# Attention with an MLP behind it: transposes one step later, inverse sums as rows through memory, first weights ahead of the last sums

## The chip, the cores and the metric

One core of a Trainium2 chip. The metric is device time of one execution in microseconds (us), the median of three runs: 931.72 before the change (931.66 to 932.09).

## What is computed

```python
q_pool = q.reshape(B, H, S // 2, 2, D).mean(axis=3)      # B 4, H 8, S 1152, D 64
scores = matmul(q_pool, k.transpose(0, 1, 3, 2)) / sqrt(D)
scores = scores - max(scores, axis=-1)
attn = exp(scores)
attn = attn / (sum(attn, axis=-1) + 1e-09)
x = matmul(attn, v)            # then to (B * S/2 tokens = 2304, H * D = 512)
h = x @ w_in                   # 512 x 2048
g = maximum(h, 0) + alpha * minimum(h, 0)
out = g @ w_out                # 2048 x 512
```

All of it in float32. The MLP's products are made of three: high by high, low by high and high by low part.

## The kernel before

**Attention.** The 32 heads are taken as 16 pairs; the two heads of a pair have 2 x 576 pooled queries, which are 9 tiles of 128 (`SOURCE`; tile 4, `MIX`, is half from either head). So there are 144 steps, one tile each, and `step` is written once for each engine; `t` is the tile's number in its pair. `over_steps` runs the first steps out by hand, then seven loop bodies of 18 steps (two pairs), then the rest. A step s does, in the order of each engine's own queue:

- PE: 16 small transposes (L587) of the first 1024 key columns of tile s's exponentials into two banks, `slot_ps`; the big scores of tile s+2 (L532, 1024 key columns); the ninth transpose (L547, the last 128 key columns) and the small scores of tile s+2 (L520), both in the middle bank of `s_ps`; then a part of the product with v (L573), of 2 to 6 matmuls. The product is made in two groups of tiles (`GROUPS`: 320 columns of tiles 0 to 4, 256 of tiles 5 to 8) and spread over later steps (`PRODUCT`). In step 6 and in step 1 a spread stands ahead of the product.
- ACT: exponential of the cut 128 columns of tile s+1 (L341), copy of slot 0 into `pt` (L357), exponential of the other 1024 columns of tile s+1 (L348). Both exponentials write their row sums, which shows as an accumulator read behind them.
- DVE: copy of slot 1 (L465), copy of the ninth block (L472), row maximum of tile s+2 (L432). In steps 4 and 8 it inverts the row sums of a group (`INVERT`), in steps 0 and 5 it scales a group's product by them (L440), and in step 5 it casts the pair's x to its high part (L446), from which POOL makes the low part (L287).
- SP: loads of q, k and v two pairs ahead, each behind a semaphore that says that its buffer is free. POOL sums pairs of q rows.

What the engines wait for in a step: PE's transposes for the exponential of tile s (`exp_done`) and for both slots (`slot_free`); the ninth transpose for its copy-out (`ninth_free`) and for the cut exponential of tile s+1 (`exp_cut_done`), which reads the same bank; DVE's ninth copy and row maximum for the small scores (`bank2_ready`, `s_ready`); ACT's cut exponential for the row maximum.

The row sums lie one query a partition, and the product has its queries along the columns. `spread_inverse` gets them there on PE: a matmul of the inverse, broadcast over 64 columns, with the identity writes it as a row into 64 partitions, piece by piece into slot 0:

```python
last[h] = nc.tensor.matmul(to[h * D:(h + 1) * D, col[h]:col[h] + m],
                           inv_sum[:, t:t + 1].to_broadcast([P, D]),
                           ident[:, first:first + m], start=True, stop=True)
```

ACT copies that to `inv_bc` (L363) and frees the slot.

**MLP.** Three passes over 768 tokens each, in two halves h of 384; 16 blocks f of 128 hidden units a pass. `hidden_unit` is 12 matmuls (L617), `output_unit` 9 (L632), in two halves in turn: hidden(f, 1), output(f, 0), hidden(f+1, 0), output(f, 1). Between them DVE forms the sum g of a half in two instructions (L479, L482), ACT casts it to its high part (L404, L415), DVE subtracts for the low part (L488). ACT casts the weights, POOL subtracts for theirs (`wi_split`, `wo_split`), SP loads them. `x_hi` and `x_lo` hold all of x in both parts. The first hidden unit comes before the last pair's second product group and its spread.

## Time and profile before

| | before |
|---|---|
| median of 3 runs | 931.72 us |
| the profiled execution | 932.26 us, its span 929.70 us |
| PE, busy of the span | 887.3 us (95%) |
| PE weight loads | 623.2 us (67%) |
| DVE | 516.9 us (56%) |
| ACT | 423.4 us (46%) |
| POOL | 213.3 us (23%) |
| attention, first step to the MLP's first matmul | 19.6 to 515.9 us |
| MLP | 515.9 to 929.7 us |

Busy shares are means over both stages. Matmuls are pipelined and their ends are modelled, so a row of PE can be busy while PE waits; starts are what they are. A span is counted from the first instruction to the last; the execution's own time has 2.56 us around it.

### The profile page before, as it was taken

Reading aid. Unit: us, or ns where it says so; the run is one execution under the profiler, and the core shown is the slowest. Engines: PE = TensorE matmul, PEld = TensorE weight load, DVE = VectorE, ACT = ScalarE, POOL = GpSimd, SP = SyncE. Lnnn points to the kernel's source line nnn. Section 1 sums busy time; section 2 is a strip of 40 time slices with the busy share of each in tenths; the row PEclk is TensorE's granted clock in tenths of the full one; section 3 lists DMA queues with packets and bytes.
Section 4 is the critical chain, followed back from the end, with each engine's and each line's share of the span. In section 5 each row is a group of like instructions: output and inputs, shape, how many; then the busy total and the mean of one; then the engine's idle time right before and its main releaser. Section 6 shows DMA issues by size and latency. Waiting matters only on the chain. (4 is left out here: it accounts for less than half of the span.)

```text
span 929.7 us, 20770 instructions
## 1 busy us (share of the span) xinstructions
PE 887.3 (95%) x6896; PEld 623.2 (67%) x6896; DVE 516.9 (56%) x836; ACT 423.4 (46%) x963; POOL 213.3 (23%) x182
## 2 busy tenths in 40 slices
PE   3799999999999999999999999999999999999997
PEld 1455555555555555555545799989999999989995
DVE  2676767677767776767676344344444444343442
ACT  2566666666666666666666222222322222322222
POOL 2112111211121112111200323323232323323230
PEclk9999999999999999999999999999999999999999
DMA  7435423542354235523520122212422222322211
GB/s 186 106 83 135 119 65 82 133 121 63 82 133 123 60 82 133 127 57 82 133 71 1 59 68 58 67 62 63 136 57 68 57 68 61 132 59 66 65 36 68
DMA packets 36366, 79.57 MB, mean 86 GB/s; under 512 B 5360, under 2 KB 9456, under 8 KB 36336
## 3 DMA queue, kind: packets, MB, share of 16 engines
q1 hardware_dynamic: 33936, 74.48, 31.0%
q10 hardware_dynamic: 2400, 4.72, 1.5%
q8 instruction: 16, 0.26, 0.1%
q14 instruction: 14, 0.11, 0.0%
HBM read 74.46 MB, written 4.72 MB: 85 GB/s over the span
## 5 line engine op out<-in xcount | busy, mean ns | idle before, releaser
L432 DVE TENSOR_REDUCE neg_max<-s_ps 128x1 f32<-128x1152 f32 x144 | 194.1, 1348 | 16.6 <-DVEq L431 16.6
L573 PE MATMUL pv_ps<-pt,v_f 128*64 128x256 f32 (+1 forms) x1152 | 169.0, 414 | 0.0
L532 PE MATMUL s_ps<-k_f,q_f 64*128 64x512 f32 (+1 forms) x640 | 160.2, 626 | 5.2 <-PEq L543 5.2
L348 ACT ACTIVATE e_sb<-s_ps,neg_max 128x1024 f32<-128x1024 f32 x144 | 160.1, 1112 | 0.0
L587 PEld LDWEIGHTS slot_ps<-ident,e_sb 64*128 64x128 f32 x2304 | 86.0, 139 | 82.4 <-issue 82.4
L465 DVE COPY pt<-slot_ps 128x512 f32<-128x512 f32 x144 | 99.6, 692 | 61.3 <-DVEq L464 59.4
L341 ACT ACTIVATE e_sb<-s_ps,neg_max 128x128 f32<-128x128 f32 x144 | 52.9, 367 | 171.5 <-ACTq L340 171.5
L617 PE MATMUL slot_ps<-x_hi,wi_hi 128*128 128x384 f32 x384 | 129.5, 337 | 1.1 <-PEq L613 1.1
L617 PE MATMUL slot_ps<-x_lo,wi_hi 128*128 128x384 f32 x384 | 129.5, 337 | 0.0
L617 PE MATMUL slot_ps<-x_hi,wi_lo 128*128 128x384 f32 x384 | 129.0, 336 | 0.0
L479 DVE TENSOR_SCALAR e_sb<-slot_ps,alpha_sb 128x384 f32<-128x384 f32 x96 | 59.3, 618 | 123.2 <-DVEq L477 123.2
L587 PE MATMUL slot_ps<-ident,e_sb 64*128 64x64 f32 x2304 | 103.5, 229 | 18.6 <-PEq L582 15.4
L488 DVE TENSOR_TENSOR g_lo<-e_sb,g_hi 128x384 fp32r<-128x384 f32 x96 | 53.7, 559 | 99.6 <-DVEq L487 99.6
L573 PEld LDWEIGHTS pv_ps<-pt,v_f 128*64 128x64 f32 x1152 | 73.5, 136 | 40.1 <-issue 0.2
L632 PE MATMUL s_ps<-wo_lo,g_hi 128*128 128x512 f32 x240 | 95.1, 396 | 0.0
L632 PE MATMUL s_ps<-wo_hi,g_lo 128*128 128x512 f32 x240 | 94.8, 395 | 0.0
L547 PEld LDWEIGHTS s_ps<-ident,e_sb 128*128 128x128 f32 x144 | 19.9, 138 | 111.5 <-issue 111.4
L632 PE MATMUL s_ps<-wo_hi,g_hi 128*128 128x512 f32 x240 | 93.4, 389 | 1.1 <-PEq L629 1.1
L303 POOL TENSOR_TENSOR wo_lo<-wo_raw,wo_hi 128x512 fp32r<-128x512 f32 x48 | 61.9, 1290 | 138.5 <-POOLq L302 138.5
L272 POOL TENSOR_TENSOR q_raw<-q_raw 128x576 f32<-128x576 f32 x32 | 45.0, 1406 | 209.7 <-POOLq L271 209.7
L404 ACT ACTIVATE g_hi<-e_sb 128x384 fp32r<-128x384 f32 x48 | 25.3, 526 | 148.9 <-ACTq L403 148.9
L295 POOL TENSOR_TENSOR wi_lo<-wi_raw,wi_hi 128x512 fp32r<-128x512 f32 x48 | 61.8, 1287 | 135.6 <-POOLq L294 135.6
(46 smaller groups left out, 1098.8 us busy)
## 6 DMA issues: line engine op xcount, KB each, us to landing
q_raw<-in_q SPq DMA_DIRECT2D x64, 288.0 KB, 4.5
k_f<-in_k SPq DMA_DIRECT2D x64, 288.0 KB, 4.2
wi_raw<-in_w_in SPq DMA_DIRECT2D x48, 256.0 KB, 2.6
wo_raw<-in_w_out SPq DMA_DIRECT2D x48, 256.0 KB, 2.6
v_f<-in_v SPq DMA_DIRECT2D x32, 288.0 KB, 3.0
out<-pt ACTq DMA_DIRECT2D x6, 768.0 KB, 4.4
k_end<-in_k SPq DMA_DIRECT2D x64, 32.0 KB, 4.0
alpha_sb<-in_alpha SPq DMA_DIRECT2D x1, 8.0 KB, 4.7
```

The lines of the kernel that those rows point to most:

```text
L295: nc.gpsimd.tensor_tensor(wi_lo[i][:, :], wi_raw[i][:, :], wi_hi[i][:, :].bitcast(F32), ALU.subtract).then_inc(pool_self, 1)
L303: nc.gpsimd.tensor_tensor(wo_lo[i][:, :], wo_raw[i][:, :], wo_hi[i][:, :].bitcast(F32), ALU.subtract).then_inc(pool_self, 1)
L348: nc.scalar.activation(e_sb[:, b * NKEY + at:b * NKEY + at + n], s_ps[:, S_AT[b] + at:S_AT[b] + at + n], ACT.Exp, bias=neg_max[:, b:b + 1] ...
L432: nc.vector.tensor_reduce(out=neg_max[:, b:b + 1], in_=s_ps[:, S_AT[b]:S_AT[b] + NKEY], op=ALU.max, axis=AX_X, negate=True).then_inc(max_r ...
L465: nc.vector.tensor_copy(pt_half(t, 1), half_columns(slot_ps[1][:, :])).then_inc(slot_free[1], 1)
L479: nc.vector.tensor_scalar(neg_sb, hid, 0.0, alpha_sb[:, bass.ds(f, 1)], ALU.min, ALU.mult).then_inc(dve_self, 1)
L488: nc.vector.tensor_tensor(g_lo[h][:, :], g_sb, g_hi[h][:, :].bitcast(F32), ALU.subtract).then_inc(g_split, 1)
L532: ins = nc.tensor.matmul(s_ps[to:to + m, S_AT[b] + at:S_AT[b] + at + BANK], q_f[2 * g + h][rows, first:first + m], k_f[2 * g + h][rows, at ...
L573: ins = nc.tensor.matmul(pv_ps[h * D:(h + 1) * D, 0:n], v_f[2 * g + h][:, a, :], pt[:, a, at:at + n], start=(a == 0), stop=(a == KT - 1))
L587: ins = nc.tensor.transpose(slot_ps[i][:, a * HALF:(a + 1) * HALF], e_sb[rows, at:at + P], ident[rows, rows])
L617: ins = nc.tensor.matmul(slot_ps[h][:, 0:TOK], w[i][:, d * P:(d + 1) * P], x[:, at:at + TOK], start=(d == 0 and w is wi_hi and x is x_hi), ...
L632: ins = nc.tensor.matmul(y_ps[h][t], g[h][:, t * P:(t + 1) * P], w[i][:, :], start=(first == 0 and j == 0), stop=(last == 1 and j == 2))
```

## The change

1. *Transposes.* Step s transposes tile s-1 (the 16 small ones and the ninth) instead of tile s. The exponentials get a third buffer in `e_sb`. PE's wait for `exp_done` stands now behind the transposes, ahead of the big scores, and the waits ahead of the ninth transpose are `exp_cut_done` first, `ninth_free` second. One step is added at the end. `PRODUCT` and `INVERT` move one step later.
2. *Inverse sums.* `spread_inverse` goes. PE transposes the [128 x 5] or [128 x 4] inverses into 5 or 4 rows in the middle bank (`turn_inverse`, in steps 6 and 1, between ninth transpose and small scores), DVE copies them to `inv_row` (between ninth copy and row maximum), SP stores them to a tensor `sums` in device memory and, when that has landed, loads them with a broadcast into 64 partitions twice, to `inv_bc`. DVE scales in steps 1 and 6, the first thing in its step. The order of queries in a pair changes so that the rows come in one piece (`SOURCE`, `SUM_AT`, `PT_AT`).
3. *x.* DVE writes the scaled product to `x_f`, all of x in float32. High and low parts are made for a half pass: the first two by POOL (`x_split`) before the MLP, the others at the end of a pass by ACT (`x_high`) and DVE (`x_low`).
4. *Weights.* The first cast of w_in stands in ACT's last step but one, ahead of the last slot copy; SP loads the first four weight blocks before it stores and spreads the last pair's sums.

The core of the diff:

```diff
 def step(s, pair, left=2):                      # PE
-    pe.wait_ge(exp_done, 1).then_inc(exp_done, -1)
-    for i in range(2):
-        pe.wait_ge(slot_free[i], 1).then_inc(slot_free[i], -1)
-    for a in range(2 * CH):
-        at = s % 2 * NKEY + a * P
+    if s > 0:
+        for i in range(2):
+            pe.wait_ge(slot_free[i], 1).then_inc(slot_free[i], -1)
+        for a in range(2 * CH):
+            at = (s - 1) % 3 * NKEY + a * P
...
+    if left >= 0:
+        pe.wait_ge(exp_done, 1).then_inc(exp_done, -1)
     if left > 1:
         begin_scores(s + 2)
         for ins in big_scores(s + 2):
             ins.then_inc(s_ready, 1)
-    pe.wait_ge(ninth_free, 1).then_inc(ninth_free, -1)
     if left > 0:
         pe.wait_ge(exp_cut_done, 1).then_inc(exp_cut_done, -1)
-    ins = transposed(s, 2 * CH, NINTH)
+    if s > 0:
+        pe.wait_ge(ninth_free, 1).then_inc(ninth_free, -1)
+        ins = transposed(s - 1, 2 * CH, NINTH)
+    if t in TURN and (TURN[t] == 0 or pair is not None):
+        ins = turn_inverse(TURN[t])
     if left > 1:
         ins = small_scores(s + 2)
     ins.then_inc(bank2_ready, 1)
...
-        if t in SPREAD:
-            pe.wait_ge(slot_free[0], 1).then_inc(slot_free[0], -1)
-            spread_inverse(SPREAD[t], slot_ps[0])
...
+def turn_inverse(group):
+    a, b = GROUP_TILES[group]
+    pe.wait_ge(inv_ready, 1).then_inc(inv_ready, -1)
+    return nc.tensor.transpose(INV_ROW[0:b - a, :], inv_sum[:, a:b], ident[:, :])
...
+def sums_and_qk(pair, g):                       # SP
+    store_sums(0)
+    load_q(pair * 2)
+    spread_sums(0)
+    sp.wait_ge(k_free[g], 1).then_inc(k_free[g], -1)
+    load_k(pair * 2, 2 * g), load_k(pair * 2 + 1, 2 * g + 1)
+    store_sums(1)
+    load_q(pair * 2 + 1)
+    spread_sums(1)
...
+def store_sums(group):
+    a, b = GROUP_TILES[group]
+    sp.wait_ge(inv_row_ready, 1).then_inc(inv_row_ready, -1)
+    sp.dma_start(sums[a * P:b * P].rearrange("(t p) -> t p", p=P),
+                 inv_row[0:b - a, :]).then_inc(inv_stored, 16)
+def spread_sums(group):
+    _, _, n, first = GROUPS[group]
+    sp.wait_ge(inv_stored, 16).then_inc(inv_stored, -16)
+    for h in range(2):
+        row = sums[GROUPS[group][h]:GROUPS[group][h] + n]
+        sp.dma_start(inv_bc[h * D:(h + 1) * D, first:first + n],
+                     row.rearrange("(o n) -> o n", o=1).to_broadcast([D, n])).then_inc(inv_bc_in[group], 16)
...
 def hidden(f, i, first, last):                  # ACT, end of a pass
     act.wait_ge(g_ready, 1).then_inc(g_ready, -1)
     nc.scalar.activation(g_hi[0], g_sb, ACT.Copy).then_inc(g_hi_done, 1)
+    if last and not last_pass:
+        x_high(n + 1, 0)
...
 def hidden(f, i, first, last):                  # DVE
     unit(f, 0)
     if n == 0 and not first:
-        scale(1)
-        x_high(NPAIR - 1)
+        scale(1, NPAIR - 1)
+    if last and not last_pass:
+        x_low(0)
     unit(f, 1)
+    if last and not last_pass:
+        x_low(1)
```

How the instructions move. First PE's queue in steps 0 and 1 of a pair, inside the loop (L587 and L631 are the small transposes, L532 and L586 the big scores, L547 and L601 the ninth transpose, L520 and L574 the small scores, L573 and L617 the product; L557 the spread, L606 the new transpose of the inverses). Before:

```order
L587 MATMUL slot_ps<-ident,e_sb 128x64 [waits exp_done,slot0_free,slot1_free]
L587 MATMUL slot_ps<-ident,e_sb 128x64 x15
L532 MATMUL s_ps<-k_f,q_f 128x512 x2
L547 MATMUL s_ps<-ident,e_sb 128x128 [waits ninth_free,exp_cut_done]
L520 MATMUL s_ps<-k_end,q_f 128x128
L557 MATMUL slot_ps<-ident,inv_sum 64x128 [waits slot0_free,inv_ready]
L557 MATMUL slot_ps<-ident,inv_sum 64x128 x3
L573 MATMUL pv_ps<-pt,v_f 64x256 x4
```

After:

```order
L631 MATMUL slot_ps<-ident,e_sb 128x64 [waits slot0_free,slot1_free]
L631 MATMUL slot_ps<-ident,e_sb 128x64 x15
L586 MATMUL s_ps<-k_f,q_f 128x512 [waits exp_done]
L586 MATMUL s_ps<-k_f,q_f 128x512
L601 MATMUL s_ps<-ident,e_sb 128x128 [waits exp_cut_done,ninth_free]
L606 MATMUL s_ps<-ident,inv_sum 4x128 [waits inv_ready]
L574 MATMUL s_ps<-k_end,q_f 128x128
L617 MATMUL pv_ps<-pt,v_f 64x256 [waits pv_free]
L617 MATMUL pv_ps<-pt,v_f 64x256 x3
```

The wait for the exponential has moved from the transposes to the big scores, the two waits ahead of the ninth transpose have changed places, and one transpose with a wait of its own stands where the spread's four matmuls stood behind the small scores (of the step before and after the same number, 1).

On DVE, step 6 after (L479 is the scale, L506 and L513 slot and ninth copy, L496 the copy of the inverse rows, L471 the row maximum); before, step 6 had L465, L472 and L432 alone:

```order
L479 ISA [waits inv_bc1_in,pv_done]
L479 TENSOR_TENSOR x_f<-pv_ps,inv_bc 128x256
L506 COPY pt<-slot_ps 128x8x64 [waits x_self,tr1_ready]
L513 COPY pt<-s_ps 128x128 [waits bank2_ready]
L496 COPY inv_row<-s_ps 5x128
L471 TENSOR_REDUCE neg_max<-s_ps 128x1 [waits s_ready]
```

The scale heads the step, and its wait holds the copies and the maximum behind it.

On SP, the first group of loads for a later pair after (L217 and L218 load q, L221 k, L237 stores the inverse rows, L246 loads them spread); before, the q and k loads stood there alone:

```order
L237 DMA sums<-inv_row 5x128 [waits inv_row_ready]
L217 DMA q_raw<-in_q 64x1152 [waits q_raw_free]
L218 DMA q_raw<-in_q 64x1152
L246 DMA inv_bc<-sums 64x320 [waits inv_stored]
L246 DMA inv_bc<-sums 64x320
L221 DMA k_f<-in_k 64x1152 [waits k0_free]
```

The loads of q stand between the store and the spread, and those of k behind both waits.

## Rows read from the trace of the kernel before

**Rows 1.** Windows by stage: us, busy us (x instructions) per engine, clock, DMA share, GB/s
```profile
19.60:52.60 33.00, 27.07 (x264) 14.54 (x263) 21.91 (x32) 19.01 (x46) 6.23 (x6) 0.95 0.53 128
52.60:485.20 432.60, 419.87 (x4274) 224.57 (x4272) 305.45 (x476) 273.62 (x658) 75.72 (x68) 1.00 0.40 99
485.20:515.90 30.70, 27.87 (x296) 15.22 (x294) 19.65 (x33) 19.62 (x46) 2.70 (x3) 1.00 0.00 1
515.90:929.70 413.80, 407.02 (x2060) 366.85 (x2060) 167.42 (x290) 108.34 (x208) 123.85 (x96) 1.00 0.24 70
```

**Rows 2.** List of waits, PE: us in total, times, longest us
```profile
PE slot_ps L587 <- PEq L582: 15.4, 35, 1.4
```

**Rows 3.** Timeline, PE: transposes of steps 0-3, 6-8, 0: start us, length us
```profile
299.77 0.71 PE L587 MATMUL slot_ps<-ident,e_sb 64*128 64x64 f32 x16
302.83 0.71 PE L587 MATMUL slot_ps<-ident,e_sb 64*128 64x64 f32 x16
306.59 0.71 PE L587 MATMUL slot_ps<-ident,e_sb 64*128 64x64 f32 x16
309.75 0.71 PE L587 MATMUL slot_ps<-ident,e_sb 64*128 64x64 f32 x16
...
319.69 0.71 PE L587 MATMUL slot_ps<-ident,e_sb 64*128 64x64 f32 x16
323.57 0.71 PE L587 MATMUL slot_ps<-ident,e_sb 64*128 64x64 f32 x16
326.84 0.71 PE L587 MATMUL slot_ps<-ident,e_sb 64*128 64x64 f32 x16
330.65 0.71 PE L587 MATMUL slot_ps<-ident,e_sb 64*128 64x64 f32 x16
```

**Rows 4.** Timeline: end of step 4's exponential and its transposes
```profile
312.62 0.21 ACT L348 ACTIVATION_READ_ACCUMULATOR e_sb<-s_ps,neg_max 128x1 f32 x1
313.27 0.71 PE L587 MATMUL slot_ps<-ident,e_sb 64*128 64x64 f32 x16 [0.35 <-PEq L582]
```

**Rows 5.** Timeline: one turn of the ninth block, step 2 to step 3
```profile
308.25 0.33 PE L547 MATMUL s_ps<-ident,e_sb 128*128 128x128 f32 x1
309.11 0.29 DVE L472 COPY pt<-s_ps 128x128 f32<-128x128 f32 x1 [0.96 <-DVEq L471]
309.32 1.35 DVE L432 TENSOR_REDUCE neg_max<-s_ps 128x1 f32<-128x1152 f32 x1
...
310.79 0.37 ACT L341 ACTIVATE e_sb<-s_ps,neg_max 128x128 f32<-128x128 f32 x1 [1.70 <-ACTq L340]
311.05 0.19 ACT L341 ACTIVATION_READ_ACCUMULATOR e_sb<-s_ps,neg_max 128x1 f32 x1
311.39 0.30 PE L547 MATMUL s_ps<-ident,e_sb 128*128 128x128 f32 x1
312.06 0.29 DVE L472 COPY pt<-s_ps 128x128 f32<-128x128 f32 x1 [0.72 <-DVEq L471]
```

**Rows 6.** Timeline, PE: the spread of step 1
```profile
304.95 0.66 PE L557 MATMUL slot_ps<-ident,inv_sum 128*64 128x128 f32 x8
```

**Rows 7.** Timeline, DVE: scale and slot copy of step 5
```profile
317.00 0.41 DVE L440 TENSOR_TENSOR x_sb<-pv_ps,inv_bc 128x256 f32<-128x256 f32 x1
317.86 0.69 DVE L465 COPY pt<-slot_ps 128x512 f32<-128x512 f32 x1 [0.44 <-DVEq L464]
```

**Rows 8.** DMA issues: count, KB each, median us from issue to landing
```profile
q_raw<-in_q SPq DMA_DIRECT2D x64, 288.0 KB, 4.5
wi_raw<-in_w_in SPq DMA_DIRECT2D x48, 256.0 KB, 2.6
```

**Rows 9.** Timeline: one MLP sum on DVE, with ACT's cast
```profile
525.12 0.62 DVE L479 TENSOR_SCALAR e_sb<-slot_ps,alpha_sb 128x384 f32<-128x384 f32 x1 [1.15 <-DVEq L477]
526.80 0.53 ACT L415 ACTIVATE g_hi<-e_sb 128x384 fp32r<-128x384 f32 x1 [5.69 <-ACTq L414]
527.48 0.56 DVE L488 TENSOR_TENSOR g_lo<-e_sb,g_hi 128x384 fp32r<-128x384 f32 x1 [1.03 <-DVEq L487]
```

More of the change, by code:

```diff
@@ L13, with build @@
 BANK = 512
-def build(nc, q, k, v, w_in, w_out, alpha, out):
+def build(nc, q, k, v, w_in, w_out, alpha, sums, out):
     HEADS, D, NKEY = k.shape
@@ L138, in build @@
         inv_ready = sem("inv_ready")
[L139 to L140 removed]
+        inv_row_ready = sem("inv_row_ready")
+        inv_stored = sem("inv_stored")
+        inv_bc_in = [sem(f"inv_bc{i}_in") for i in range(2)]
         pv_done = sem("pv_done")
         pv_free = sem("pv_free")
[L143 removed]
+        x_done = sem("x_done")
         x_hi_done = sem("x_hi_done")
@@ L178, in over_steps, with x_chunk, x_part @@
                     step(s, two * 2)
-            for s in range(FIRST, REST):
+            for s in range(FIRST, REST + 1):
                 step(s, 2 * BODIES, REST - 1 - s)
+        def x_chunk(n, h):
+            at = (2 * n + h) * TOK
+            return x_f[:, :].rearrange("p (d c) -> p d c", d=DT)[:, :, at:at + TOK]
+        def x_part(part, h):
+            return part[h].rearrange("p (d c) -> p d c", d=DT)
         def pt_half(t, half):
-            at = PT_AT[t] if half == 0 else PT_MIX if t == MIX else PT_AT[t] + HALF
+            at = PT_AT[t] + half * HALF
             return pt[:, 0:2 * CH, at:at + HALF]
@@ L443, in scale @@
                 dve.sem_inc(pv_free, 1)
-            def x_high(pair):
-                nc.vector.tensor_copy(x_hi[:, bass.ds(pair * NQ, NQ)], x_sb[:, :]).then_inc(x_hi_done, 1)
+                if group == 1:
+                    dve.sem_inc(x_done, 1)
             def invert(group):
@@ L507, in hidden @@
                     if n == 0 and not first:
-                        scale(1)
-                        x_high(NPAIR - 1)
+                        scale(1, NPAIR - 1)
+                    if last and not last_pass:
+                        x_low(0)
                     unit(f, 1)
+                    if last and not last_pass:
+                        x_low(1)
                 over_hidden(dve, hidden)
@@ L603, in step, with hidden_unit @@
                 group, tiles = PRODUCT[t]
-                if group == 0 or pair is not None:
-                    if t in SPREAD:
-                        pe.wait_ge(slot_free[0], 1).then_inc(slot_free[0], -1)
-                        spread_inverse(SPREAD[t], slot_ps[0])
-                    product(group, g if group == 0 else 1 - g, tiles)
-            def hidden_unit(n, f, i, h):
+                if t > 5:
+                    product(group, g, tiles)
+                elif pair is not None:
+                    product(group, 1 - g, tiles)
+            def hidden_unit(n, f, i, h, first):
+                if not first:
+                    pe.wait_ge(x_ready, 1).then_inc(x_ready, -1)
                 if h == 0:
```

238 lines of the change are left out of this document (115 added, 123 removed).

## The prediction

> **What bounds the kernel now.** I read the windows by stage first [rows 1]. From 515.90 us on, in the MLP, PE is busy 407.02 of 413.80 us at a granted clock of 1.00: nothing but fewer columns could help there. The fourteen head pairs from 52.60 to 485.20 us take 432.60, so 30.90 us for a pair of nine steps; PE shows 419.87 busy, but its matmul ends are modelled, and I trust starts instead. The list of waits [rows 2] says where PE stands: 35 times before the transposes L587, 15.4 us. So I took the starts of the transposes in one pair [rows 3, 4]: the steps last 3.06, 3.76, 3.16, 3.52, then 6.42 for two, 3.88, 3.27 and 3.81 us.
>
> What PE itself needs follows from these. Step 8 has two product matmuls of 320 columns more than step 7 and takes 0.54 more: 0.27 each, 0.215 for 256 columns. Step 7 less four of them is 2.19, and 2.19 plus four of 256 is 3.05, which is step 0. These three steps are PE's alone. Step 3 should then be 3.06 and is 3.52, and steps 4 and 5 should be 2.62 and 3.27 and are together 0.53 more. Steps 1 and 6 hold the spread of the inverses.
>
> Two things stop PE. **The exponential**: the accumulator read of step 4's exponential ends at 312.62+0.21 = 312.83, and the transposes start at 313.27, 0.44 later [rows 4]; three waits stand before them. **The ring of the ninth block** [rows 5], one turn a step: ninth transpose at 308.25, ninth copy on DVE 0.86 later (0.67 where the tile is from one head: 311.39 to 312.06), row maximum 0.21 later for 1.35, the cut exponential on ACT 0.12 later, its accumulator read ending 0.45 after that (311.24), next ninth transpose 0.15 later at 311.39. That is 3.14 us, and 2.95 for an ordinary tile: hardly under PE's 3.05.
>
> **The change, part by part.**
> *Spread out.* Ten matmuls a pair go, each shown as two records. The twelve records of step 6 add 3.88-3.27 = 0.61; the eight of step 1, 0.66 us in the trace with a modelled end [rows 6], should add two thirds of that, 0.41. Step 1 has another 3.76-3.05-0.41 = 0.30 of waiting: its next transposes wait for ACT's copy out of the slot.
> *Transposes one step later.* They no longer wait for an exponential. The wait stands now between them and the big scores, and is early: from a cut exponential's start to the end of the big one's read are 312.83-310.79 = 2.04 us [rows 4, 5], so it is done 0.67+0.21+1.35+0.12+2.04 = 4.4 us after the ninth transpose that let it start, while the scores that need it begin two turns later less their own 1.0, over 5.1. I cost it at nothing; its cover is 0.7 us. The 0.47 of step 3 and 0.53 of steps 4 and 5 go with it. What is late next is the ring.
> *The ring gets longer.* The two waits before the ninth transpose are turned round: the cut exponential's comes first, then one for ninth_free. Three waits give 0.44 [rows 4], the last of two gives 0.15 [rows 5], so an already satisfied wait behind the late one costs (0.44-0.15)/2 = 0.15. Bounds: 0, as PE may have read ahead, and 0.29. I take 0.15: 3.10, and 3.29 for the mixed tile. The Trainium skill ("Advanced Engine Details and Errata", Miscellaneous Facts) gives 50 to 100 ns for reading a semaphore from a sequencer; with 0.10 the sum below would be near 3 us lower. The rows decide.
> *Turn and rows, in steps 1 and 6.* Between ninth transpose and small scores come a wait and a 128-column transpose: 0.15 + 0.66/8 = 0.23. Before the row maximum DVE copies the row out, at the 0.21 pitch of the ninth copy. No trace shows either; below, PE's queue hides both (0), above 0.29+0.15 and a whole 0.45. With them the ring is 3.10+0.23+0.21 = 3.54.
> *Products one step later.* No column more; the six-matmul step is now step 0, the two-matmul step 5.
>
> From ninth transpose to ninth transpose, the larger of PE and ring: 0 to 1: 3.81 (2.19+6x0.27); 1 to 2: 3.54; 2 to 3: 3.29; three times 3.10 (PE would need 3.05, 3.05, 2.62); 6 to 7: 3.54; 7 to 8 and 8 to 0: 3.27. Sum 30.02 against 30.90: 0.88 a pair, **13.2 us** over 15 pairs.
>
> *DVE.* Scale and its two waits move into steps 1 and 6. In step 6 the previous row maximum ends 2.2 us after ninth transpose 5, scale takes 0.41 and, from its start to the slot copy's, 0.86 (of which before the change a part is waiting), the copy 0.69 [rows 7]: 3.75, and the next ninth copy is due at 3.10+0.23+0.67 = 4.0. Just hidden. The cast x_high leaves DVE, ACT's two row copies a pair leave ACT: no gain beyond what is counted.
> *SP.* Per pair two stores and four spreads enter the queue, with waits, past q, k and v loads. The spread is due when DVE reaches scale: from step 6 to step 1, 3.54+3.27+3.27+2.2, less 1.1 until the row is out: 11.2 us. Needed: landing, two issues of 0.6, landing. With 2.6 (weights) or 4.5 (q) for a landing [rows 8], 6.4 to 10.2. Hidden; k loads start about 2 us later, with tens of us to spare.
> *Start.* Steps 0 to 5 have no product and hung on both waits; the first pair takes 33.00 [rows 1]. At the ring's pace it loses most of the excess: 2 us, between 0 and 4.
> *End of attention.* One step more (transposes and ninth, 0.8) but without the wait for the last exponential and for the first weights: PE's idle time is 30.70-27.87 = 2.83 [rows 1]. I take 0, between -1.5 and +1.
> *First MLP sums.* Spread out, turn in: -0.3. Scale of the last group now waits for store and spread: the row is out 3.3 us after the MLP's first matmul, spread landed near 9.4, scale and first sum (2.92 from its start to the end of g_lo [rows 9]) give 13.2, PE wants it at 12.6: +0.6, between 0 and 5. The Trainium skill ("DMA: Bandwidth & Descriptors", Anatomy of one DMA) puts the fixed part of a DMA near 2.0 us; by that the 0.6 would be 0.
> *Splits of x.* POOL's first two splits lie beside the last steps, where POOL is busy 2.70 of 30.70 us [rows 1]; hidden. At the two pass boundaries ACT casts 1536 columns (0.53 for 384, so about 1.4) and DVE subtracts 1536 (0.56 for 384, about 1.8) twice [rows 9], in DVE's order between sums that fill 2.92 of every 4.19 us. Let hidden unit 15 of half 0 end at 0. Cast ends 3.8, subtract 5.8; the second sum starts at 5.85 and not 4.5, its g_lo reaches PE at 8.91, wanted 8.37: 0.54. Second subtract ends 11.3, wanted 11.0: 0.48. Then the next pass's first sum is ready at 14.46, wanted 13.57: 0.89. So 1.9 a boundary, **3.8 us** for two; below 0 if PE's slack is larger, above 6.
>
> Sum: -13.2 -2.0 +0 -0.3 +0.6 +3.8 = -11.1. The profiled execution took 932.26 (span 929.70), 0.54 above the median of the runs; 921.2 against it, 920.7 as a median.
>
> **Rivals.**
> *The waits are free.* PE reads ahead, and the reordered wait and the turn's wait cost nothing. For: the k and q waits stand between transposes and scores in steps 7 and 8, and those steps are not longer than PE needs. Against: the 0.44 [rows 4]. Ring 2.95, 3.24 with turn and row: 3.81+3.24+3.16+3.05+3.05+2.95+3.35+3.27+3.27 = 29.15, a gain of 26 instead of 13: 908.
> *Handoffs eat it.* The ring takes 0.29 for the wait, and turn and row 0.6: 3.24 in three steps, 3.43, 3.84 twice, sum 31.0. Then pairs are as long as now, start and boundaries cancel: 930 to 934. It needs both upper bounds.
> *The round trip is late* (slower). DVE's queue stops at scale if the spread has not landed; copies, maxima and ninth blocks stand behind it. It decides from 11.2 us for the trip, that is landings over 5.0 us each; the q load just before the spread is for it, the 4.5 of the longest loads against [rows 8]. The ring has no slack to win it back: each us over costs 1 a pair, 15 in all; landings of 6 us give 2 over, 30 less 13: 947.
> *The change does not do what it says*: the transposes still wait. The queue order excludes it but for the slot copies, which end before the next product does.
>
> **Chances.** Forecast 0.52 (914 to 927), free waits 0.24 (905 to 914), no net gain 0.10, late trip 0.08, other trouble, such as DVE over its 0.25 of cover in step 6, 0.06. A measurement tells 0.2% (1.9 us) from no change. Faster 0.80, same 0.05, slower 0.15. The range, 907 to 930, leaves out the bottom of the second case, the late trip and the worst of the rest.
>
> **What would show it.** Starts of the transposes 30.0 us a pair; no wait before them, and PE's waits now before the ninth transpose (its line in the list of waits) in steps 2 to 6; 0.29 or 0.15 from accumulator read to ninth transpose tells the first rival from the forecast. DVE's scale must not be the longest wait in steps 1 and 6. Two pauses of PE near 1.9 us at the pass boundaries. A pair of over 30.9 us, or a trip over 11 us, would make me wrong.

## The result and the profile after

The changed kernel takes 916.3 us (median of 4 runs, 915.69 to 916.85) against 931.7 us before: 15.4 us less, ratio 0.9835 (95% interval 0.9818 to 0.9852). The forecast was 920.7, in a range from 907 to 930. The profiled execution's span is 913.9 us against 929.70, so the two traces differ by 15.8.

The windows by stage of the changed kernel, cut at the same steps as [rows 1] (a step begins with its first transposes, which now belong to the step before). The columns are those of [rows 1].

```profile
19.60:49.60 30.00, 25.43 (x223) 12.70 (x221) 20.05 (x29) 17.89 (x44) 5.56 (x5) 1.00 0.55 128
49.60:466.00 416.40, 406.18 (x4022) 209.98 (x4020) 305.99 (x491) 258.93 (x630) 64.89 (x59) 1.00 0.45 110
466.00:497.00 31.00, 29.42 (x307) 15.58 (x305) 21.12 (x38) 19.20 (x45) 3.62 (x3) 1.00 0.19 64
497.00:913.90 416.90, 408.33 (x2055) 365.95 (x2053) 174.15 (x295) 113.54 (x211) 126.24 (x95) 1.00 0.23 70
```

Stage by stage: the first pair 33.00 to 30.00, the fourteen pairs 432.60 to 416.40 (30.90 to 29.74 a pair), the end of attention 30.70 to 31.00, the MLP 413.80 to 416.90. The pairs and the start give the gain, as forecast; the end of attention gives nothing (its window holds more work than before, see below), and the MLP takes 3.1 us back.

The list of waits for PE of the changed kernel (us in total, times, longest):

```profile
PE s_ps L601 <- PEq L645: 13.8, 38, 0.9
...
PE s_ps L682 <- PEq L679: 2.0, 4, 1.1
PE slot_ps L666 <- PEq L663: 0.8, 2, 0.4
```

The line of [rows 2] is gone: no transpose of a block waits any more. So the change does what it says, and that rival is out. In the line's place stands the ninth transpose, L601, 38 times: the ring. The last two lines are the MLP's output and hidden units at the pass boundaries, but for 1.1 us of the second, which stands ahead of the last output unit and stood there before the change too.

One turn of the ring with turn and row in it, step 1 to step 2 of a pair, from the timeline of the changed kernel (start, length), to be read against [rows 5]:

```profile
322.77 0.33 PE L601 MATMUL s_ps<-ident,e_sb 128*128 128x128 f32 x1
...
322.93 0.27 PE L606 MATMUL s_ps<-ident,inv_sum 128*4 128x128 f32 x1
...
323.04 0.39 PE L574 MATMUL s_ps<-k_end,q_f 128*128 128x128 f32 x2
...
323.58 0.29 DVE L513 COPY pt<-s_ps 128x128 f32<-128x128 f32 x1 [0.48 <-DVEq L511]
323.79 0.27 DVE L496 COPY inv_row<-s_ps 4x128 f32<-4x128 f32 x1
323.99 1.33 DVE L471 TENSOR_REDUCE neg_max<-s_ps 128x1 f32<-128x1152 f32 x1
...
325.71 0.19 ACT L377 ACTIVATION_READ_ACCUMULATOR e_sb<-s_ps,neg_max 128x1 f32 x1
...
326.19 0.30 PE L601 MATMUL s_ps<-ident,e_sb 128*128 128x128 f32 x1
```

The turn delays the small scores by 0.11 us (322.93 to 323.04) and the row copy delays the row maximum by 0.20 (323.79 to 323.99). From the cut exponential's read (325.71+0.19 = 325.90) to the next ninth transpose are 0.29, where [rows 5] had 0.15.

From ninth transpose to ninth transpose, means over 13 pairs, against the forecast's table (these are my means of the starts in the timeline):

| turn | before | forecast | changed | e1_order | e5_lag_only |
|---|---|---|---|---|---|
| 0 to 1 | 3.07 | 3.81 | 3.81 | 3.81 | 3.81 |
| 1 to 2 | 3.88 | 3.54 | 3.43 | 3.28 | 3.83 |
| 2 to 3 | 3.14 | 3.29 | 3.26 | 3.13 | 3.28 |
| 3 to 6, three turns | 9.87 | 9.30 | 9.31 | 9.06 | 9.39 |
| 6 to 7 | 3.88 | 3.54 | 3.41 | 3.36 | 3.92 |
| 7 to 8, 8 to 0 | 7.07 | 6.54 | 6.51 | 6.54 | 6.54 |
| a pair | 30.90 | 30.02 | 29.72 | 29.18 | 30.76 |

### The profile page after: what moved, and what is told of

Same layout as the page of the kernel before. It is cut to its first block and busy times, and to the rows that moved or that the text cites. A ratio compares the mean times of both kernels' runs of the same rounds, so it can differ in the third digit from the quotient of the medians.

```text
span 913.9 us, 20102 instructions
## 1 busy us (share of the span) xinstructions
PE 875.2 (96%) x6608; PEld 606.6 (66%) x6608; DVE 523.8 (57%) x856; ACT 412.4 (45%) x935; POOL 205.1 (22%) x170
## 5 line engine op out<-in xcount | busy, mean ns | idle before, releaser
L666 PE MATMUL slot_ps<-ff 128*128 128x384 f32 x1152 | 218.0, 337 | 0.8 <-PEq L663 0.8
L666 PEld LDWEIGHTS slot_ps<-ff 128*128 128x128 f32 x1152 | 204.3, 188 | 11.1 <-issue 3.1
L471 DVE TENSOR_REDUCE neg_max<-s_ps 128x1 f32<-128x1152 f32 x144 | 193.7, 1345 | 18.0 <-DVEq L470 18.0
L682 PE MATMUL s_ps<-ff 128*128 128x512 f32 x720 | 182.4, 394 | 2.0 <-PEq L679 2.0
L617 PE MATMUL pv_ps<-pt,v_f 128*64 128x256 f32 (+1 forms) x1152 | 169.8, 417 | 0.0
L586 PE MATMUL s_ps<-k_f,q_f 64*128 64x512 f32 (+1 forms) x640 | 159.6, 630 | 5.7 <-PEq L597 5.1
L682 PEld LDWEIGHTS s_ps<-ff 128*128 128x128 f32 x720 | 133.4, 188 | 26.5 <-issue 3.6
L631 PEld LDWEIGHTS slot_ps<-ident,e_sb 64*128 64x128 f32 x2304 | 83.6, 139 | 60.7 <-issue 60.2
L506 DVE COPY pt<-slot_ps 128x512 f32<-128x512 f32 x144 | 99.5, 691 | 33.2 <-DVEq L505 29.2
L531 DVE TENSOR_TENSOR ff<-e_sb,ff 128x384 fp32r<-128x384 f32 x96 | 53.7, 559 | 99.9 <-DVEq L530 99.9
L601 PEld LDWEIGHTS s_ps<-ident,e_sb 128*128 128x128 f32 x144 | 19.9, 138 | 127.7 <-issue 127.5
L631 PE MATMUL slot_ps<-ident,e_sb 64*128 64x64 f32 x2304 | 103.2, 230 | 0.0
L617 PEld LDWEIGHTS pv_ps<-pt,v_f 128*64 128x64 f32 x1152 | 71.0, 136 | 45.2 <-issue 0.3
L337 POOL TENSOR_TENSOR ff<-wi_raw,ff 128x512 fp32r<-128x512 f32 x48 | 64.0, 1333 | 156.9 <-POOLq L336 156.9
L345 POOL TENSOR_TENSOR ff<-wo_raw,ff 128x512 fp32r<-128x512 f32 x48 | 64.1, 1335 | 141.8 <-POOLq L344 141.8
L439 ACT ACTIVATE ff<-e_sb 128x384 fp32r<-128x384 f32 x48 | 25.3, 526 | 153.8 <-ACTq L438 153.8
L513 DVE COPY pt<-s_ps 128x128 f32<-128x128 f32 x144 | 42.0, 292 | 85.0 <-DVEq L511 83.2
L452 ACT ACTIVATE ff<-e_sb 128x384 fp32r<-128x384 f32 x48 | 25.2, 526 | 144.0 <-ACTq L451 144.0
```

The lines of the kernel that those rows point to most:

```text
L337: nc.gpsimd.tensor_tensor(wi_lo[i], wi_raw[i][:, :], wi_hi[i].bitcast(F32), ALU.subtract).then_inc(pool_self, 1)
L345: nc.gpsimd.tensor_tensor(wo_lo[i], wo_raw[i][:, :], wo_hi[i].bitcast(F32), ALU.subtract).then_inc(pool_self, 1)
L471: nc.vector.tensor_reduce(out=neg_max[:, b:b + 1], in_=s_ps[:, S_AT[b]:S_AT[b] + NKEY], op=ALU.max, axis=AX_X, negate=True).then_inc(max_r ...
L506: nc.vector.tensor_copy(pt_half((s - 1) % TILES, 1), half_columns(slot_ps[1][:, :])).then_inc(slot_free[1], 1)
L531: nc.vector.tensor_tensor(g_lo[h], g_sb, g_hi[h].bitcast(F32), ALU.subtract).then_inc(g_split, 1)
L586: ins = nc.tensor.matmul(s_ps[to:to + m, S_AT[b] + at:S_AT[b] + at + BANK], q_f[2 * g + h][rows, first:first + m], k_f[2 * g + h][rows, at ...
```

## The experiments

Twelve kernels ran, in four groups; the kernel before took 931.1 to 931.7 us beside each. Each is the changed kernel with the edit shown, but for e7_both, e11_hold and e10_held, which start from e1_order. The edits are cut to their main lines.

**Which wait costs.** The forecast charged 0.15 us a turn for a satisfied wait behind the late one, and its first rival nothing. Three kernels touch only the waits before the ninth transpose.

e1_order, the order turned back:

```diff
+                if s > 0:
+                    pe.wait_ge(ninth_free, 1).then_inc(ninth_free, -1)
                 if left > 0:
                     pe.wait_ge(exp_cut_done, 1).then_inc(exp_cut_done, -1)
                 if s > 0:
-                    pe.wait_ge(ninth_free, 1).then_inc(ninth_free, -1)
                     ins = transposed(s - 1, 2 * CH, NINTH)
```

> Only the two waits ahead of the ninth transpose change places (ninth_free first, the cut exponential's last, as before the change). Theory (a satisfied wait behind the late one costs 0.15 us in the ring of the ninth block): accumulator read of the cut exponential to ninth transpose 0.15 instead of 0.30 us; the ring-bound turns 3 to 4, 4 to 5 and 5 to 6 go from 3.10 to 3.05, 3.05 and 2.95, turn 1 to 2 from 3.43 to 3.28, 2 to 3 from 3.26 to 3.14; a pair from 29.72 to 29.2 us, the whole about 8 us shorter than the changed kernel, 908. Rival (where the wait stands is free, and the 3.10 has another cause): a pair stays at 29.7 and the time at 916.

Measured: 906.98 us, ratio 0.9741 (0.9724 to 0.9757), 9.3 us under the changed kernel; 29.18 a pair.

e2_extra_wait adds `pe.wait_ge(always, 1)` after ninth_free, without the decrement that the other waits have; e2b_counting_wait adds `pe.wait_ge(always, 1).then_inc(always, -1)`.

> The changed kernel with one more wait behind the other two ahead of the ninth transpose, on a semaphore that is set at the start and never taken down. Theory: another 0.15 us in the ring, if a wait that does not count down costs what one that does costs: turns 3 to 6 at 3.25 instead of 3.10, 1 to 2 at 3.57, 2 to 3 at 3.41; steps 7, 8 and 0 are PE's own and stay; a pair about 30.5, the whole 12 us longer, 928. If a wait costs half of that (0.07): 922. Rival (waits are free): 916.

Measured: 916.46 us, ratio 0.9842 (0.9825 to 0.9858), 29.72 a pair: nothing. My theory missed here, and the next run asks whether the decrement is what costs.

> Changed kernel with one more wait before the ninth transpose on a semaphore that is always filled, and this one counts down by one as the real waits do. The wait of the run e2_extra_wait did not count down and cost nothing. Theory (a satisfied wait that counts down behind the late one costs PE about 0.15 us): read to ninth transpose 0.45 instead of 0.30, the turns of steps 3 to 5 at 3.25, and the ring's others longer by the same, 6 of 9: 30.6 us a pair, near 929 us. Rival (any satisfied wait is free, and the order of the two waits matters for another reason): 29.72 a pair and 916 us as the changed kernel.

Measured: 930.27 us, ratio 0.9986 (0.9976 to 0.9996), 30.63 a pair; turns 3 to 6 are 3.25 each. One more counting wait eats nearly the whole gain of the change. The last read and the ninth transpose after it, from the timelines of e1_order, e2_extra_wait and e2b_counting_wait, in this order:

```profile
302.75 0.19 ACT L377 ACTIVATION_READ_ACCUMULATOR e_sb<-s_ps,neg_max 128x1 f32 x1
...
303.09 0.30 PE L601 MATMUL s_ps<-ident,e_sb 128*128 128x128 f32 x1 [0.29 <-PEq L645]
```

```profile
302.94 0.19 ACT L378 ACTIVATION_READ_ACCUMULATOR e_sb<-s_ps,neg_max 128x1 f32 x1
...
303.43 0.30 PE L603 MATMUL s_ps<-ident,e_sb 128*128 128x128 f32 x1
```

```profile
304.31 0.19 ACT L378 ACTIVATION_READ_ACCUMULATOR e_sb<-s_ps,neg_max 128x1 f32 x1
...
304.95 0.30 PE L603 MATMUL s_ps<-ident,e_sb 128*128 128x128 f32 x1 [0.24 <-PEq L648]
```

From the read's end: 0.15, 0.30 and 0.45 us. With the late wait last there is 0.15; each counting wait behind it adds 0.15; one that does not count down adds nothing. In step 3 of the 13 pairs of the table the gap is 0.14 to 0.15 in e1_order, 0.29 to 0.30 in the changed kernel and in e2_extra_wait, and 0.45 in e2b_counting_wait. That is the forecast's mechanism and value; what it left out is that the price hangs on the decrement. Why the decrement costs is not shown, and the plain wait was tried only as the last in the list.

**What the lag and the rows are worth apart.** e3_exp_first keeps all but puts the wait for exp_done back ahead of the (late) transposes. e4_rows_no_lag keeps the turn, row copies, stores and spreads, but takes the transposes of the step itself, with PRODUCT, INVERT, TURN and SCALE one step earlier. e5_lag_only keeps the lag and puts the spread by matmuls and ACT's copies back.

```diff
                 t, g = s % TILES, s // TILES % 2
+                if left >= 0:
+                    pe.wait_ge(exp_done, 1).then_inc(exp_done, -1)
                 if s > 0:
                     for i in range(2):
...
-                if left >= 0:
-                    pe.wait_ge(exp_done, 1).then_inc(exp_done, -1)
                 if left > 1:
                     begin_scores(s + 2)
```

> The changed kernel with PE's wait for the big exponential of tile s put back ahead of the transposes, which still are those of tile s-1. Theory: the exponential is done 4.4 us after the ninth transpose that let it start, then 0.44 to the transposes and 1.58 to the next ninth transpose: two turns take at least 6.4 us, where 2 to 6 now take 3.26 and three times 3.10. So about 0.3 to 0.5 us a pair, 5 to 8 us in all: 921 to 924. Rival (the lag is what gives the time, whatever the wait): all of the lag's part is lost and the time goes to 925 or more. Rival (the wait never counts): 916.

Measured: 924.90 us, ratio 0.9931 (0.9914 to 0.9948), 30.20 a pair. The ninth transpose of step 10 starts at 57.09, where the changed kernel has 54.95: the gain at the start is gone too. 0.48 for each of 14 pairs and 2.1 once are 8.8, for the 8.6 measured.

Of the 2.1 us, 1.7 are there by the ninth transpose of step 3 (33.45 for 31.74), and the wait alone is not what they are made of. PE in the timeline of e3_exp_first, and one of its windows (the third value from its end is the granted clock):

```profile
30.64 1.06 PE L633 MATMUL slot_ps<-ident,e_sb 64*128 64x64 f32 x16 [1.06 <-PEq L628]
31.44 2.08 PE L586 MATMUL s_ps<-k_f,q_f 64*128 64x512 f32 x4
```

```profile
32.00:34.00 2.00, 2.00 (x7) 0.56 (x3) 0.54 (x1) 1.46 (x3) 0.00 (x0) 0.50 0.26 80
```

PE stood for 1.06 us and then ran at 0.50 of its clock, the lower level (1.2 GHz): from the big scores to the ninth transpose 2.01 us (31.44 to 33.45), for 1.01 in a steady step of the changed kernel (321.76 to 322.77). The granted clock of the changed kernel is 1.00 there.

```diff
-                if t in TURN and (TURN[t] == 0 or pair is not None):
-                    ins = turn_inverse(TURN[t])
...
+                if t in TURN and (TURN[t] == 0 or pair is not None):
+                    pe.wait_ge(slot_free[0], 1).then_inc(slot_free[0], -1)
+                    spread_inverse(TURN[t], slot_ps[0])
```

(The first cut is of e3_exp_first, the second of e5_lag_only, PE's part. e4_rows_no_lag puts the minus lines of the change's own diff of `step` back, with the third buffer of `e_sb`, and the tables PRODUCT, INVERT, TURN and SCALE one step earlier.)

> The changed kernel without the lag: transposes of tile s in step s with the old order of waits, products, inversions, turns and scales one step earlier; inverse sums still by turn, store and spread. Theory by the rings (two turns at least 6.4 us, turn and row 0.33 once in each half, PE's 3.27, 3.27 and 3.81 for steps 6, 7 and 8): a pair near 29.9 to 30.0 us, so that the rows alone give about 0.9 of the 1.18 us a pair, and the whole takes 919 to 922. Rival (the lag is the main part): a pair near 30.5, the whole near 928.

Measured: 923.35 us, ratio 0.9917 (0.9900 to 0.9933), 30.20 a pair, 0.2 over my theory. The list of waits for PE of e3_exp_first, then of e4_rows_no_lag:

```profile
PE slot_ps L633 <- PEq L628: 16.0, 35, 1.2
```

```profile
PE slot_ps L626 <- PEq L621: 20.1, 52, 1.5
```

Both again wait before the transposes, 16.0 and 20.1 us in all against 15.4 in [rows 2]. e3_exp_first differs from the changed kernel by the place of one wait, so that place is worth 0.48 a pair. That both pairs are 30.20 long does not show that the later transposes bought nothing by themselves: e4_rows_no_lag has the old order of the two waits before the ninth transpose and e3_exp_first the new one, and the turns differ both ways (2 to 3: 3.30 in e3, 3.13 in e4; 3 to 6: 9.67 and 9.87). With the old order on both sides, e4_rows_no_lag against e1_order, lag and moved wait together are worth 1.02 a pair (30.20 to 29.18).

> Changed kernel with the lagged transposes, but the inverse sums spread on PE as before (ten matmuls a pair, copied out of the slot by ACT); no store, no spread by transfers. Theory (lag and rows each act by themselves: the lag takes the wait for the exponential from steps 3 to 5 and 2 us from the start, the spread still costs PE 0.41 in step 1 and 0.61 in step 6, and in step 1 the transposes still wait 0.30 for the copy out of the slot): turns 3.81, 3.76, 3.29, 3.10, 3.10, 3.10, 3.88, 3.27, 3.27, together 30.58 us a pair, 0.9 more than the changed kernel, so near 929 us. Rival (with the transposes late there is no more wait behind the spread, or the spread fits into the time in which PE waits for the ring): 29.9 us a pair or less, near 919. Second rival (the lag is worth nothing without the rows): 30.9 and 932 or more.

Measured: 932.61 us, ratio 1.0010 (1.0000 to 1.0019), 30.76 a pair: the second rival. My turns were close (30.58), only 0.14 of the 0.32 came, and the boundaries take 3.4 us back. The timeline of its step 1:

```profile
302.77 0.33 PE L578 MATMUL s_ps<-ident,e_sb 128*128 128x128 f32 x1
...
304.06 0.38 ACT L379 ACTIVATE inv_bc<-slot_ps 128x256 f32<-128x256 f32 x1 [0.33 <-ACTq L378]
...
304.92 0.71 PE L617 MATMUL slot_ps<-ident,e_sb 64*128 64x64 f32 x16 [0.15 <-PEq L612]
```

The slot holds the spread until ACT has copied it out, and the transposes start 2.15 us after the ninth transpose; in the changed kernel they start 1.60 after it (322.77 to 324.37). So the lag gives little while the spread is there: rows alone 0.70 a pair, lag alone 0.14, both 1.18. These three are not quite alike, since e4_rows_no_lag has the old order of the two waits and the other two the new one; the lag alone with the old order was not run.

**The weights ahead of the last sums.** e8_late_cast moves ACT's wi_high(0) back behind the last slot copy.

```diff
-                elif left == 0:
-
-                    wi_high(0)
...
-            wi_high(1), wo_high(0)
+            wi_high(0), wi_high(1), wo_high(0)
```

> Changed kernel with the cast of the first weight block on ACT put back behind the last slot copy (the move of the first MLP weights ahead of the last sums undone); all else as changed. Theory (by the trace of the changed kernel PE's first hidden matmul would wait for cast and split, about 0.7 us): 916.5 to 917.5 us, PE waits before the first hidden matmul. Rival (the move bought the whole of the end of attention): 918 or more. Second rival (it bought nothing): 916.3.

Measured: 917.47 us, ratio 0.9847 (0.9831 to 0.9864), 1.2 over the changed kernel. Its timeline:

```profile
498.71 2.32 PE L663 MATMUL slot_ps<-ff 128*128 128x384 f32 x12 [1.08 <-PEq L660]
```

PE waits 1.08 us for the split that now comes late; this part of the change is worth about 1.1 us.

**The pass boundaries.** In the changed kernel the units of PE around a boundary (2.09 us each elsewhere) last 2.22, 2.37, 2.73, 2.68 and 2.15 at the first, 1.7 too long in all, and they are 1.7 too long at the second: 3.4 us. The timeline of the first:

```profile
631.07 1.76 DVE L553 TENSOR_TENSOR ff<-x_f,ff 128x1536 fp32r<-128x1536 f32 x1 [0.82 <-DVEq L552]
...
631.62 2.36 POOL L345 TENSOR_TENSOR ff<-wo_raw,ff 128x512 fp32r<-128x512 f32 x1 [4.27 <-POOLq L344]
632.75 0.61 DVE L522 TENSOR_SCALAR e_sb<-slot_ps,alpha_sb 128x384 f32<-128x384 f32 x1
...
638.53 2.32 PE L666 MATMUL slot_ps<-ff 128*128 128x384 f32 x12 [0.42 <-PEq L663]
```

e7_both is e1_order with the splits cut in pieces: VectorE's subtract in halves, one of them in the pause in which it waits for g_hi; ACT's second cast ahead of its g; PE waits twice a unit.

```diff
-                        x_low(0)
-                    unit(f, 1)
-                    if last and not last_pass:
-                        x_low(1)
+                        x_low(n + 1, 0, 0)
+                    unit(f, 1, (lambda: x_low(n + 1, 0, 1)) if split else None, split)
+                    if split:
+                        x_low(n + 1, 1, 0)
```

> The run e1_order (the wait for ninth_free first, the one for the cut exponential last; 906.98 us) and besides, at the two pass boundaries of the MLP, the splits of x in smaller pieces: the subtract on DVE in halves of 768 columns (one of them in the time in which DVE waits for g_hi), the second cast on ACT ahead of its g, PE waits for the second half only when it comes to it. Nothing left out. Theory (the 3.3 us at the boundaries are waits behind whole splits in DVE's order): up to 3.3 us of them come back, 903.7 to 905 us. Rival (DVE's and ACT's time there is what is short, however it is cut): 907 as e1_order, or above by the added instructions.

Measured: 905.94 us, ratio 0.9727 (0.9711 to 0.9743): 1.0 of the 3.4. Two units of PE at each boundary remain long, 2.53 and 2.89 at the first. The timeline of e7_both shows what lies between them:

```profile
625.14 1.32 POOL L338 TENSOR_TENSOR ff<-wi_raw,ff 128x512 fp32r<-128x512 f32 x1 [1.66 <-POOLq L337]
625.23 2.05 DVE L561 TENSOR_TENSOR ff<-x_f,ff 128x768 fp32r<-128x768 f32 x1
```

VectorE's 768 columns take 2.05 us where the same piece elsewhere takes 0.96: its subtract began 0.09 after GpSimd's and ends 0.82 after that one's end. That can be behind the second long unit only. The first, from 623.58, waits in its middle for a piece of x that took its usual 0.96 and ended at 624.84, before the two subtracts met: its 0.44 us belong to where the pieces are cut. e11_hold was to turn the order round, by a semaphore that VectorE raises after its piece and GpSimd waits for.

> The run e7_both (905.94 us) with one thing more: at each pass boundary GpSimd's subtract for the next w_in block waits until VectorE has begun its first half of the second split of x. In e7_both GpSimd began that subtract 0.09 us ahead of VectorE, and VectorE's 768 columns took 2.05 us instead of 0.96. Theory (a subtract of one of the two engines holds off the other's until it is done, whichever began first): VectorE's piece takes 0.96 again, GpSimd's takes about 2 us instead of 1.3 at no cost, and 0.6 to 0.8 us a boundary come back: 904.3 to 904.8 us. Rival (the two engines share SBUF's bandwidth and both slow down): VectorE's piece stays near 2 us, 905.9.

Measured: 905.13 us, ratio 0.9719 (0.9703 to 0.9736), but the trace shows that the edit did not do what it should: GpSimd still begins at 624.73, VectorE at 624.82 and for 2.05 us, the units are 2.53 and 2.89 again. The signal came before the subtract had begun. This run tells nothing of the theory, and its 0.8 us under e7_both lie within the spread of the two kernels' runs (904.61 to 906.10 and 905.26 to 906.23).

e10_held cuts the pieces otherwise, [0, 3, 4] and [0, 2, 3, 4] quarters, with e11_hold's semaphore:

```diff
+    PIECES = [(0, 3, 4), (0, 2, 3, 4)]
...
+                    unit(f, 0, (lambda: (x_low(n, 1, 1), x_low(n, 1, 2))) if n > 0 and not first else None)
```

> As e11_hold, and the splits of x cut otherwise: three quarters of the first half ahead of the last sum and the last quarter in its pause for g_hi; of the second half two quarters ahead of the next sum and one and one in its pause; PE waits for each piece where it comes to it. Theory (with the right order VectorE's time suffices, each deadline being met within 0.1 us): both boundaries cost under 0.5 us together, 903.5 to 904 us. Rival (VectorE's time at the boundary is what is short, however cut): no better than e11_hold.

Measured: 903.80 us, ratio 0.9704 (0.9687 to 0.9720), the fastest of all, 12.5 us under the changed kernel. No unit of PE at either boundary is over 2.15 us. The timeline of e10_held:

```profile
625.28 0.95 DVE L565 TENSOR_TENSOR ff<-x_f,ff 128x768 fp32r<-128x768 f32 x1
625.37 2.03 POOL L340 TENSOR_TENSOR ff<-wi_raw,ff 128x512 fp32r<-128x512 f32 x1 [1.66 <-POOLq L339]
```

Here VectorE is 0.09 ahead, and now GpSimd's takes 2.03 instead of 1.3. So e10_held shows by its order what e11_hold could not. It changes order and cut at once, and no run separates them; by the long units of e7_both at the first boundary the cut could give back 0.44 us and the order 0.80.

**The turn.** e12_turn_twice makes the small transpose twice.

```diff
+                nc.tensor.transpose(INV_ROW[0:b - a, :], inv_sum[:, a:b], ident[:, :])
                 return nc.tensor.transpose(INV_ROW[0:b - a, :], inv_sum[:, a:b], ident[:, :])
```

> Changed kernel (916.3 us) with the turn of the inverse sums made twice, the second time to the same place and with no wait of its own. Theory (a turn costs its columns on the ring, 0.11 us, and the wait before it, long satisfied, costs next to nothing): the two ring turns 1 to 2 and 6 to 7 grow from 3.43 and 3.41 by 0.08 to 0.11, 0.2 a pair, 3 us in all: 919.3 us. Rival of the forecast's sizing (the 0.11 was all wait, the columns hide in PE's queue): no change, 916.3. Second rival (a turn is 0.23, as forecast, and something else gave 0.12 back): 0.46 a pair, 923.

Measured: 919.66 us, ratio 0.9869 (0.9853 to 0.9886), 29.95 a pair, 0.23 more; the turns 1 to 2 and 6 to 7 grow by 0.10 and 0.11. From its timeline:

```profile
325.15 0.27 PE L606 MATMUL s_ps<-ident,inv_sum 128*4 128x128 f32 x1
...
325.26 0.27 PE L607 MATMUL s_ps<-ident,inv_sum 128*4 128x128 f32 x1
...
325.37 0.39 PE L574 MATMUL s_ps<-k_end,q_f 128*128 128x128 f32 x2
```

Each is 0.11 to the next. A turn costs 0.11. The counting wait before it costs nothing that shows: in the changed kernel the turn starts 0.16 after the ninth transpose (322.77 to 322.93), and in plain steps the small scores start 0.14 to 0.16 after it (329.45 to 329.59, 318.96 to 319.12 in its timeline).

**The round trip.** e13_long_trip stores the row four more times, one after the other, before each spread.

```diff
+                for again in range(4):
+                    sp.wait_ge(inv_stored, 16).then_inc(inv_stored, -16)
+                    sp.dma_start(sums[a * P:b * P].rearrange("(t p) -> t p", p=P),
+                                 inv_row[0:b - a, :]).then_inc(inv_stored, 16)
                 sp.wait_ge(inv_stored, 16).then_inc(inv_stored, -16)
```

> Changed kernel with the round trip of the sums made longer: before each spread the row is stored four more times, each store issued when the one before has landed. By the trace of the changed kernel the trip takes about 6.4 us from the row copy's end to the landing of the spread, and is due 13.7 us after it in step 1 to 6 and 11.2 us after it in step 6 to 1; a store takes 1.5 to 1.8 from issue to issue, so four take 6 to 7 and the trip 12.5 to 13.5. Theory (the forecast's third rival is right in its mechanism and its point, 11.2 us, and only the trip was short): the scale in step 1 waits 1.3 to 2.3 us, nothing wins it back, pairs of 31.0 to 32.0, 936 to 951 us, and the scale of the last group holds the first MLP sums too. Rival (PE's queue and the slots absorb a late scale): under 0.5 a pair, 916 to 924.

Measured: 941.24 us, ratio 1.0086 (1.0060 to 1.0112), 30.97 a pair. In its timeline the row is out at 322.38+0.27 = 322.65 and the scale starts 13.0 us later:

```profile
335.65 0.49 DVE L484 TENSOR_TENSOR x_f<-pv_ps,inv_bc 128x320 f32 x1 [2.10 <-DVEq L483]
```

Of the 25 us more, 17.5 are 14 pairs of 1.25. The rest comes at the MLP's start, where the last scale waits 7 us. The windows of e13_long_trip there (columns as in [rows 1]; the eighth value is the granted clock):

```profile
524.60:526.70 2.10, 2.10 (x11) 1.72 (x10) 0.00 (x0) 0.00 (x0) 0.00 (x0) 1.00 0.04 11
526.70:528.80 2.10, 2.10 (x13) 1.95 (x11) 0.22 (x1) 0.00 (x0) 0.00 (x0) 1.00 0.71 186
528.80:532.50 3.70, 0.18 (x2) 0.03 (x1) 2.08 (x5) 1.04 (x2) 0.15 (x1) 0.90 0.66 208
532.50:536.50 4.00, 4.00 (x10) 3.13 (x11) 1.50 (x3) 0.52 (x1) 1.13 (x1) 0.50 0.24 66
536.50:539.50 3.00, 3.00 (x13) 3.00 (x12) 0.00 (x0) 0.63 (x1) 1.28 (x1) 0.66 0.00 0
```

PE stands from 528.8 to 532.5, and then its granted clock is 0.50, the lower level (1.2 GHz), for 4 us and 0.66 on the mean of the next 3, so partly back at 2.4 GHz: the output unit takes 3.98 us and the hidden one 3.05, for 2.09 each. The pause of 3.7 us cost another 2.9 by the clock.

## Why the prediction was right, and where its sizes were off

**The bound: right.** The transposes' wait for the exponential went, and the ring became the bound. Its plain turn was forecast at 3.10 and is 3.10; the order of two waits carries it (e1_order: 3.02 without).

**The price of a wait: right for the ring, wrong as a rule.** I took (0.44-0.15)/2 = 0.15 from [rows 4, 5]; the three runs give 0.15 for a counting wait directly behind the late one, and not the 0.10 tried beside it (which by the forecast's own table would have made the sum 6 us lower, not near 3). But I also charged 0.15 in the turn, whose wait stands behind a running transpose: there it is 0. "The waits are free" is out (its 908 us is what the other order gives, 906.98), though its observation, that the k and q waits cost nothing in steps 7 and 8, holds for waits in PE's shadow.

**Turn and rows: mis-sized.** Forecast 0.23 + 0.21 a turn; measured 0.11 + 0.20. Of the 0.23, 0.15 was a wait that costs nothing there and 0.08 the columns, which cost 0.11. Over the two turns of a pair that is 0.24 of the 0.30 us by which the pair is shorter than forecast. "Handoffs eat it" needed 0.29 a wait and is out; e2b_counting_wait shows how near it lay. (Its table adds up to 31.18 and not 31.0, so it stood for near 3 us more than its 930 to 934 say.)

**Spread out, lag.** The forecast had no figure for either alone. e4_rows_no_lag and e5_lag_only show 0.70 and 0.14 a pair, 1.18 together. Its "I cost it at nothing" for the moved wait holds: in the list of waits of the changed kernel PE stands before the big scores only for 0.5 us in the first pair.

**Start: -2.0 forecast, right in size, its reason open.** The ninth transpose of step 10 comes 2.24 earlier, but 1.53 of that is there by step 2 (30.01 to 28.48), so the ring's pace over the steps behind it gives only 0.7. In the kernel before, PE stood for 1.35 us and then got the lower clock, from the timeline and the windows:

```profile
23.89 1.06 PE L587 MATMUL slot_ps<-ident,e_sb 64*128 64x64 f32 x16 [1.35 <-PEq L582]
```

```profile
24.00:26.00 2.00, 2.00 (x20) 1.19 (x19) 0.93 (x2) 1.44 (x4) 0.00 (x0) 0.50 0.31 44
26.00:28.00 2.00, 2.00 (x20) 1.10 (x19) 0.27 (x2) 0.71 (x2) 0.00 (x0) 0.64 1.10 279
```

The changed kernel's windows there have a clock of 1.00, although its own big scores at 23.30 take 1.95 us too. How much of the 1.53 is the clock's is not separated. The forecast gave the clock no price, though [rows 1] has 0.95 for the first pair, so the fit of the 2.0 is in part luck.

**End of attention: 0 forecast**, +0.3 by the windows, though e8_late_cast shows that the early cast is worth 1.1 us in it. The windows with PE's product alone (PE, weight loads, clock, DMA share, GB/s), before and after:

```profile
485.20:515.90 30.70, 10.65 (x74) 4.60 (x72) 1.00 0.00 1
466.00:497.00 31.00, 12.48 (x86) 5.19 (x84) 1.00 0.19 64
```

Twelve records more are six matmuls of 320 columns: those that the change moves from step 8 of a pair to step 0 of the next, so into this window from the one before. At 0.27 us each they are 1.6 us of PE's time. The extra step's transposes (0.8) and two turns (0.2) make up for the two spreads (1.0), and so PE is 1.55 us busier (29.42 for 27.87), while its pauses fell from 2.83 to 1.58. The forecast had counted the extra step's transposes and not this. At the first pair the same six matmuls have left (36 records before, 24 after), so the two windows are to be read together: 2.7 us shorter, where the forecast had 2.0 and 0.9.

**First MLP sums: -0.3 right, +0.6 absent.** The last store's spread is issued 1.24 us after the store (499.97 to 501.21), where I had taken 2.6 for the landing. The last scale starts at 504.78, 1.3 us after its product ended and still in time for PE. The Trainium skill ("DMA: Bandwidth & Descriptors", Anatomy of one DMA) puts the fixed part near 2.0 us, for transfers that GpSimd issues; by that the term would have been 0, as it is. This store, on SyncE's queue, was shorter still.

**The trip: right.** It was to decide from 11.2 us; from the row copy to the landing it takes some 6.4 us here. The timeline of the changed kernel:

```profile
324.15 0.27 SPq L237 DMA_DIRECT2D sums<-inv_row  x1
...
325.82 1.16 SPq L246 DMA_DIRECT2D inv_bc<-sums  x2
...
337.80 0.41 DVE L479 TENSOR_TENSOR x_f<-pv_ps,inv_bc 128x256 f32 x1
```

The second spread is issued by 326.98, and the median landing of a spread is 3.8 us: landed near 330.5 by that estimate, used at 337.80. e13_long_trip confirms the mechanism. Its price was forecast too high: DVE idles 1.84 us on the mean before the scale of step 1, where the changed kernel has 0.35, so it starts 1.5 late, and the turn 1 to 2 grows by 0.93 and not by 1.5, since the ninth copy behind it had 0.48 of cover (the idle time at 323.58 above). The turn 6 to 7 grows by 0.28 more. (The forecast's 947 does not come out of its terms either: 30 less 13 on 931.7 is 949.)

**Pass boundaries: 3.8 forecast, 3.4 measured,** from the three waits forecast: 0.54, 0.48 and 0.89 by my sum, 0.41 (over two units), 0.64 and 0.59, with 0.06 after it, in the trace. I had the subtract at 1.8 and the cast at 1.4; they are 1.76 and 1.47. That GpSimd's split would be pushed to 2.36 us I had not seen; PE waits nowhere for it in the changed kernel, but in e7_both the same collision stands before a unit that is 0.8 too long.

The sum: forecast -11.1, measured -15.4 in the medians and -15.8 in the spans. By the windows the fourteen pairs gave 3.9 us more than forecast (16.2 for 12.3), the MLP cost 1.0 less (3.1 for 4.1), and the start and the end of attention together gave 0.2 less (2.7 for 2.9). So the mechanism held, and the term that was mis-sized is the turn, with 0.24 us a pair by far the largest part of the error.

## What to carry to other kernels

Where a loop between engines sets the pace, put the wait that ends last in last place: here one swap of two waits was worth 9.3 us, more than half of the whole change, and each counting wait behind the late one costs the loop 0.15 us a turn. Two parts of a change that free the same slot must be priced together: here apart they gave 0.70 and 0.14, together 1.18 a pair. When a change moves work by a step, windows cut at steps no longer hold the same work. Work that moves from one engine to another should be cut to the pauses of the new one (e10_held, 2.1 us under e7_both, with the order turned as well).
